# Two score steps ahead of two first-layer groups, and causal masks by TensorE in odd halves, in a fused attention, expert and mixing kernel on one core

## The reference, cut to what matters

```python
# 1: linear attention with decay, 8 heads of 48
y[t] = r[t] @ (state + u * k[t] v[t]);  state = w[t] * state + k[t] v[t]
# 2: four attention experts of 64, two of them gated in for a token
for e in range(4):
    scores = scale * (x @ wq[e]) @ (x @ wk[e]).T
    scores = where(causal, -1e9, scores)          # the mask: keys after the query
    a = softmax(scores)
    out += gate[e] * ((a @ (x @ wv[e])) @ wo[e])
# 3: mixing; xk, xr are blends of x and x shifted by a token
k = maximum(xk @ w_k, 0)                          # 384 -> 1024, the first layer
v = k * k @ w_v
return sigmoid(xr @ w_r) * v
```

## Time and profile before

| | |
|---|---|
| median of three runs | 699.25 us (698.36 to 699.54) |
| the profiled execution, its own time | 698.35 us |
| its span | 696.6 us |
| TensorE busy | 676.7 us, 97% of the span |
| VectorE, ScalarE, GpSimd busy | 403.1, 322.5, 153.9 us |
| mean granted clock of TensorE | 0.995 |

### The profile page before, as it was taken

One profiled execution on the slowest core, in us unless ns is written; L12 is line 12 of the kernel. 1 busy time (PEld: TensorE's weight loads), 2 busy tenths in 40 slices (PEclk: granted clock), 3 DMA queues, 4 the chain that ended last, 5 costly groups with the idle time before them and its releaser, 6 DMA issues.

```text
span 696.6 us, 12285 instructions
## 1 busy us (share of the span) xinstructions
PE 676.7 (97%) x4780; PEld 444.0 (64%) x4780; DVE 403.1 (58%) x795; ACT 322.5 (46%) x805; POOL 153.9 (22%) x200
## 2 busy tenths in 40 slices
PE   7969999999999999999999999999999999999998
PEld 7856656766656665666656665666665666566554
DVE  7997996473874657637474738747477223661200
ACT  2455557622762266632655227662166314563340
POOL 7772530053201601017010522004420000000000
PEclk9998999999999999999999999999999999999999
DMA  9994500003400080000800044000000000000000
GB/s 253 315 340 154 168 23 1 1 1 115 154 0 2 24 243 2 1 1 24 243 2 1 2 121 147 1 1 1 36 0 2 1 24 11 1 1 12 23 1 34
DMA packets 36921, 43.35 MB, mean 62 GB/s; under 512 B 2560, under 2 KB 27264, under 8 KB 36608
## 3 DMA queue, kind: packets, MB, share of 16 engines
q1 hardware_dynamic: 36864, 42.57, 20.3%
HBM read 37.84 MB, written 4.72 MB: 61 GB/s over the span
## 4 chain that ended last, share of the span: by engine, by line
PE 88%; DVE 7%; ACT 2%; issue 1%; POOL 1%; DVEq 0%; POOLq 0%; ACTq 0%
PE bank L948 76%; PE bank L952 6%; PE bank L1114 3%; PE bank L1110 3%; DVE nmax L704 1%; DVE shared L717 1%; ACT shared L459 1%; DVE idec L670 1%; DVE bank L697 1%; ACT L538 1%; DVE att L737 0%; POOL rk_sb L355 0%; DVE rinv L712 0%; DVE rinv L714 0%; DVE gsum L798 0%
## 5 line engine op out<-in xcount | busy, mean ns | idle before, releaser
L948 PE MATMUL bank<-wv_sb,k_sb 128*128 128x384 f32 x384 | 139.4, 497 | 0.0
L948 PE MATMUL bank<-xk_sb,wk_sb 128*128 128x384 f32 x384 | 138.6, 500 | 0.6 <-ACT act_sb L443 0.6
L948 PEld LDWEIGHTS bank<-xk_sb,wk_sb 128*128 128x128 f32 x384 | 68.4, 189 | 50.3 <-issue 8.5
L948 PEld LDWEIGHTS bank<-wv_sb,k_sb 128*128 128x128 f32 x384 | 67.5, 190 | 38.8 <-issue 3.7
L459 ACT ACTIVATE shared<-bank,nmax 128x128 f32<-128x128 f32 (+5 forms) x96 | 60.0, 629 | 59.8 <-DVE nmax L704 59.8
L670 DVE RECIPROCAL idec<-dec 112x260 f32<-112x260 f32 x48 | 82.8, 1755 | 0.5
L386 POOL TENSOR_TENSOR state<-state,carry 112x512 f32<-112x512 f32 x20 | 22.0, 1098 | 255.8 <-DVE state L756 132.8
L948 PE MATMUL bank<-xT_sb,wqk_sb 128*128 128x384 f32 (+1 forms) x240 | 64.1, 424 | 0.6 <-ACT xT_sb L513 0.6
L496 ACT ACTIVATE att<-ident,bonus 128x128 f32<-128x128 f32 x192 | 58.0, 391 | 13.8 <-DVE bonus L678 10.8
L691 DVE TENSOR_TENSOR out_sb<-bank,sg_sb 128x384 f32<-128x384 f32 x24 | 13.4, 557 | 85.2 <-PE bank L948 84.9
L513 ACT COPY xT_sb<-bank 128x384 f32<-128x384 f32 x24 | 11.5, 479 | 100.2 <-PE bank L1114 100.2
(11 more groups left out here) (93 smaller groups left out, 933.2 us busy)
## 6 DMA issues: line engine op xcount, KB each, us to landing
rk_sb<-in_rk SPq DMA_DIRECT2D x24, 384.0 KB, 6.9
v_sb<-in_v SPq DMA_DIRECT2D x24, 256.0 KB, 7.5
w_sb<-in_wT SPq DMA_DIRECT2D x24, 227.5 KB, 4.9
r_sb<-in_rT SPq DMA_DIRECT2D x24, 224.0 KB, 5.0
k_sb<-in_kT SPq DMA_DIRECT2D x24, 224.0 KB, 5.8
out<-out_sb SPq DMA_DIRECT2D x24, 192.0 KB, 1.9
wk_sb<-in_w_k SPq DMA_DIRECT2D x1, 1536.0 KB, 11.0
wv_sb<-in_w_v SPq DMA_DIRECT2D x1, 1536.0 KB, 15.4
```

What stands on the lines that cost most here:

```text
L948: return nc.tensor.matmul(out, lhsT, rhs, start=start, stop=stop)
```

## The change

The scores of steps 0 and 1 stand side by side, with no filling between. The first-layer groups 0 and 1 stand behind both, and group 1 is written to bank 6. The third chunk of `mix_gate` goes to bank 6 too (in the last half it already did), so that bank 3 is free for the scores. For steps 0 and 1 of the odd halves, TensorE puts the mask on, by the two bf16 matmuls that half 0 uses, and VectorE's `copy_predicated` is left out. The waits follow: group 1 waits for the sigmoids in place of `relu` 0, `output` of step 0 waits for `relu` 1, and the third chunk of `mix_gate` for VectorE's copy of the first values (`proj_dve` + 3 in place of + 1).

```diff
 def mix_bank(hh, i):
     if i < FT and hh != LAST:
-        return 7
+        return 6 if i == 1 else 7
     return RING[i % 3] if hh == LAST else RING[i - FT]

 def r_bank(h, t):
-    return (4, 5, 6 if h == LAST else 3)[t]
+    return (4, 5, 6)[t]

 def fill_a(i):
-    groups = {0: ((0,), ()), 1: ((1,), ()), 2: ((), (2,)), 3: ((), (3,)), 4: ((), (4,)), 5: ((), (5,)), 6: ((6,), (7,))}[i]
+    groups = {0: ((), ()), 1: ((0, 1), ()), 2: ((), (2,)), 3: ((), (3,)), 4: ((), (4,)), 5: ((), (5,)), 6: ((6,), (7,))}[i]

+        def masked_by_pe(h, i):
+            return h == 0 or (h % 2 == 1 and i < QM)
+        def masked_until(h, i):
+            return sum(not masked_by_pe(a, x) for a in range(h + 1) for x in range(STEPS if a < h else i + 1))

     # ScalarE, attention_step
+                    if i == 1:
+                        relu(h - 1, 0)
                     exponentials(h, i)
-                    relu(h - 1, i)
                     if i >= 1:
+                        relu(h - 1, i)

     # VectorE, maxima
-                if h > 0:
+                if not masked_by_pe(h, i):
                     ...
-                    dve.wait_ge(score_masked, (h - 1) * STEPS + i + 1)
+                    dve.wait_ge(score_masked, masked_until(h, i))
                 for e in range(2):
                     n = 2 * i + e
-                    if h == 0:
-                        dve.wait_ge(score_psum, n + 1)
+                    if masked_by_pe(h, i):
+                        dve.wait_ge(score_psum, h * TILES + n + 1)

     # TensorE, mix
+                    elif hidden and i == 1:
+                        pe.wait_ge(r_ready, (hh + 1) * HC)
                     elif hidden and i > 0:
-                        pe.wait_ge(relu_ready, hh * FT + i)
+                        pe.wait_ge(relu_ready, hh * FT + (i if i > 2 else 1))

     # TensorE, score_step
-                if i == 1 and h > 0:
-                    pe.wait_ge(r_ready, h * HC)
...
-                for e in range(2 if h == 0 else 0):
+                for e in range(2 if masked_by_pe(h, i) else 0):
                     mm(scores(h, i, e)[:, q0:w], ident_b[:, :], later_b[:, :], start=False).then_inc(score_psum, 1)

     # TensorE, output
+                else:
+                    pe.wait_ge(relu_ready, (h - 1) * FT + 2)

     # TensorE, mix_gate
                     if c == 2 and h < LAST:
-                        pe.wait_ge(proj_dve, h * (QM + HC) + 1)
+                        pe.wait_ge(proj_dve, h * (QM + HC) + QM + 1)
```

More of the change, by code:

```diff
@@ L1009, in score_step @@
                         x = mm(scores(h, i, e)[:, lo:hi], qk_sb[rows, m, q0:w], qk_sb[rows, QM + m, lo:hi],
-                               stop=h > 0 or hi != w)
-                        if h > 0 and hi == w:
+                               stop=not masked_by_pe(h, i) or hi != w)
+                        if not masked_by_pe(h, i) and hi == w:
                             x.then_inc(score_psum, 1)
-                for e in range(2 if h == 0 else 0):
+                for e in range(2 if masked_by_pe(h, i) else 0):
                     mm(scores(h, i, e)[:, q0:w], ident_b[:, :], later_b[:, :], start=False).then_inc(score_psum, 1)
```

## The result

The changed kernel takes 695.62 us (median of six runs, 695.03 to 696.28), against 698.82 for the kernel before in the same session (six runs, 698.16 to 699.54): 3.2 us less, a ratio of 0.9954 (95% interval 0.9944 to 0.9964). The prediction had 1.85 us less, 697.4, and its range began at 696.2. The direction and the place were right, and the size was not.

What follows compares the result with a forecast made beforehand. The prediction took TensorE to bound the kernel almost everywhere. Half 1's 0.74, three odd halves at 0.37 and the even halves' 0 summed to 1.85 us less, a median of 697.4, range 696.2 to 699.2.

Steps and rivals of the forecast that it cites:

- the wait that took the gain: Even halves, TensorE before `output` of step 0, waiting for ScalarE: forecast to grow from 0.17 to 0.37 us.
- relu 0: Odd halves, ScalarE: relu 0 ahead of the exponentials of step 1 was to cost nothing, with 0.6 us of cover.
- the bank of the third chunk: `mix_gate`'s third chunk waits for the first values copied by VectorE: forecast cover 4.9 us, cost 0.
- the copies in the odd halves: ScalarE's copies (1.08 us) before `output` of step 0: forecast to end 0.2 us ahead, so no new wait.
- step 4: Odd halves, half 3's times: same work before the transposes, TensorE later than the chain, wait gone, 0.37 us won.
- step 3: Masks on TensorE in odd halves: 0.12 us a pair, 0.24 a half, 0.96 for eight pairs; upper bound 0.28 a pair.
- step 5: Half 1, before the scores of step 2: TensorE free at 105.23, chain at 105.26, so 0.74 us won.
- the case that the stop takes some of the gain: Half 1: if the scaling's 0.49 us wait stands still in time, only the 0.47 of step 1 is won.
- The term, 0: Even halves: ScalarE is late next, so they win 0; bounds 0 and 0.6 us for all three.
- step 6: Odd halves, ScalarE: group 0 ends at 269.13, relu 0 at about 269.75, before the first maximum of step 1 at 270.35.
- The dearer mask: Rival, odd halves: a mask pair costs 0.28 us, total gain 0.6, 698.65; chance 0.32, shared with a half chain.
- the drain of the masks: Rival, odd halves: masks drain TensorE, over 0.2% slower from 0.53 us a pair; at 0.64, +2.3 us, 701.5; chance 0.05.

## Why the prediction was right or wrong

**Right: the place and the mechanism.** The 2.83 us of waits at step 2 are gone, because VectorE's chain got shorter. The masks alone give 2.5 us and the order alone gives nothing. The even halves win nothing, and the wait that took the gain is the one that was named. No new wait came from relu 0, the bank of the third chunk, or the copies in the odd halves.

**Wrong: the size in step 4, "the wait is gone, 0.61 - 0.24 = 0.37 us are won".** Measured, 0.68 in each of halves 3, 5 and 7. Four terms of it were mis-sized, by reading records as if they were spacings, or by leaving out what neighbours lose to each other:

- *The masks' price (step 3), 0.12 a pair.* In the old order a pair costs 0.06 net, since the group behind it is 0.05 shorter. That is 0.12 in a half.
- *The transposes.* The free time of TensorE was put at 271.02 + 1.03. A record's end is later than the start of what could follow: without a wait the next row comes 0.97 after their start. The wait was 0.06 longer than its row said.
- *The scores behind the wait.* After a wait `output` follows them by 1.35 (before, half 3), without one by 1.28. That is 0.07 more.
- *The order (step 4, "the same work stands between").* The work is the same, its time is not. The order saves 0.43 (order alone), and a pair between two scores costs 0.31 more than behind both, so that the two pairs cost 0.50 in the new order (5.89 to 6.39) and 0.12 in the old one. Together with the masks the changed kernel is at the transposes after 6.39, the masks alone after 6.44: 0.06 is all that the order adds (between halves it reads as 0.05 or 0.06).

0.37 + 0.12 + 0.06 + 0.07 + 0.06 = 0.68.

One of the prediction's own signs of being wrong came true: "if a pair of masks takes over 0.2 us". The pair of step 0, which stands between two scores, takes 0.22 (265.14 to 265.36), the one of step 1 the forecast 0.12.

**Half 1 (step 5), 0.74 forecast, 0.99 measured.** In the changed kernel the last exponential has been read out at 105.27 and the scores of step 2 start at 105.32, in the same 0.05 as before (half 3 has 0.23 there). So the chain sets the start, though TensorE, 0.97 after its transposes, comes free in the same moment. The chain became 1.00 us shorter. The first exponential came 0.34 earlier, not 0.27, again since an idle time was counted from the end of a record that overlaps its neighbour. And the stop of 0.49 became one of 0.24, one instruction later. The scaling of the probabilities (L727) starts 0.71 after the end of the gate in place of 0.89, so this gave 0.18, which nothing in the prediction stood for: it had only the case that the stop takes some of the gain. 0.47 + 0.34 + 0.18 is the 1.00 within 0.01. The 0.18 was luck.

**Even halves.** The term, 0, was right: -0.06 in three. The wait was not: 0.83 to 0.89 in place of the forecast 0.3 to 0.4. The 0.40 that the side by side order saves TensorE was left out, and landed in the wait.

**Two slips in its working** change little. The sum for group 0 in step 6 gives 269.22 and not 269.13 (267.89 + 1.09 + 0.24), and the lower end of the range, 0.5 under 696.8, is 696.3 and not 696.2. Neither would have moved the forecast.

**The two rules cited.** The Trainium skill (TensorEngine Tiling, "Key Properties") has a change of tiling mode drain TensorE. The prediction found no row to tell such a drain from other spacing; the runs have one. Taking the two changes of mode out saves 0.43 us with scores 512 wide (order alone) and 0.40 with scores 128 wide (even halves in the old order against the new), so it is a fixed cost and not a share of the work: by estimate from these, some 0.2 us a change. The rule fits. Lost overlap between the two scores would read alike in part only: of the 0.43 the scores' rows save 0.23 (1.06 + 1.09 to 1.92) and the groups' rows 0.20 (2.13 + 2.04 to 3.97), and of the 0.40 they save 0.19 and 0.20. That it is a drain, and not some other loss at each border, no run shows. The Trainium skill (TensorE: Matmul & The Clock Gate, "Back-to-back issue gap") has 81 ns for a matmul of 128 columns in a stream with weight loads. These masks do not bear it out: a further pair costs 0.11 us, so 55 ns a matmul.

**The rivals.** The dearer mask (0.28) and the drain of the masks (0.53 or more) do not hold for a pair as such: 0.06 net in the old order, 0.08 to 0.12 behind both scores, 0.11 for one more. But where a pair parts two scores it costs 0.31 us more, and in the changed kernel that is paid for by what the order saves. So the dearer mask had a true part, which no row before could show, and its time was still wrong. Faster had the largest chance and came; the range was too narrow below, as nothing in it stood for terms that all erred against the gain.

## What to carry to other kernels

A wait in the list is as long as the gap between two starts less what the first takes when nothing waits behind it; take that from a row without a wait, not from the record's length, which hid 0.06 us of the wait here, and another 0.07 in the scores behind it. Ask for each instruction put onto a busy TensorE what its neighbours gain or lose: here the masks in the old order cost half their spacing, and a pair between two scores 0.31 us more than behind both. And when an order saves the bound engine time that ends in a wait, that wait shows where to look next: moving one group into it and shortening its chain brought 2.2 us.

## What was not expected of the hardware

- Scores that use half of the array's rows each, 64 deep: two steps back to back take 1.92 us for 2 * 1.06 at 512 columns and 0.64 or 0.65 for 0.42 + 0.42 at 128. The saving is about 0.2 us in both (half 3 of the order alone, half 2 before and after).
- VectorE can stand for 0.23 to 0.49 us between two small instructions with nothing outstanding that the profile shows. The place and size repeat from execution to execution (0.49 and 0.47; 0.44 and 0.44) and differ from program to program: `output` 0 of halves 4 and 6 came after 6.69 or 6.70 us in the kernel with only the mask of step 1, and after 6.46 or 6.47 in others with the masks of the even halves on VectorE and no group moved, and with the same instructions there. In half 1 the stop stayed before the same instruction, counted from the start, when one was taken out ahead of it. Its cause stays open; it is as large as the masks that were being weighed, and made one expectation wrong by 1.3 us.
